# A kernel of attention and two MoE layers: V's local windows are loaded as runs of 112 keys

## The reference

```
# q, k, v: [4 batches, 8 heads, 576 tokens, 64]
q_d, k_d, v_d = means over groups of 4 tokens            # 144 tokens
out_up    = repeat(softmax(q_d k_d^T / 8) v_d, 4)        # pooled attention
mask      = |i - j| < 4                                  # a band of 7 keys
out_local = softmax(where(mask, q k^T / 8, -1e9)) v      # local attention
x = (out_up + out_local) as [2304 tokens, 512]
x = g(x @ w_in) @ w_out,    g = h * tanh(softplus(h))    # 512 -> 2048 -> 512
x = layernorm(h * softmax(h)) @ w_out2,  h = x @ w_in2   # 512 -> 1024 -> 512
```

## Time and profile before

| What | Value |
|---|---|
| Time, median of 3 runs | 689.77 us (688.67 to 690.86) |
| Span of the profiled execution | 686.9 us |
| The same execution's time beside the span | not recorded: the span is 2.9 us under the median of the runs |
| PE busy, share of the span | 667.5 us, 97% |
| DVE busy | 425.9 us, 62% |
| ACT busy | 326.0 us, 47% |
| POOL busy | 284.2 us, 41% |
| DMA packets | 26085, of them 12714 under 2 KB |

### The profile page before, as it was taken

The page is one execution under the profiler, slowest core; times in us unless marked ns, Lnnn a source line. Parts: engine busy times, 40 slices in busy tenths (PEclk is TensorE's granted clock), DMA queues, the critical chain, the costliest instruction groups (busy, mean ns, idle before and its releaser), DMA issues.

```text
span 686.9 us, 12938 instructions
## 1 busy us (share of the span) xinstructions
PE 667.5 (97%) x5002; PEld 573.1 (83%) x5002; DVE 425.9 (62%) x747; ACT 326.0 (47%) x687; POOL 284.2 (41%) x342
## 2 busy tenths in 40 slices
PE   6998899999999999999999999999999999999998
PEld 5777778888999989989899988888778888888886
DVE  7998759555765557555544412555788566766671
ACT  5998773233543446543443211137464454535441
POOL 6999713020694636645000000576435543354100
PEclk9999999999999999999999999999999999999999
DMA  8999692000000000000100001012100000000001
GB/s 259 247 262 262 157 336 114 0 1 1 0 1 1 1 1 1 1 1 1 62 1 2 1 0 35 27 31 63 31 17 16 31 32 31 8 25 31 32 16 46
DMA packets 26085, 37.52 MB, mean 55 GB/s; under 512 B 2484, under 2 KB 12714, under 8 KB 26026
## 3 DMA queue, kind: packets, MB, share of 16 engines
q1 hardware_dynamic: 26026, 36.71, 18.0%
HBM read 31.98 MB, written 4.72 MB: 53 GB/s over the span
## 4 chain that ended last, share of the span: by engine, by line
PE 89%; POOL 3%; DVE 2%; issue 2%; ACT 1%; DMA 1%; SPq 0%; POOLq 0%; DVEq 0%
PE psum L961 29%; PE psum L913 16%; PE psum L1074 13%; PE psum L1051 12%; PE psum L947 12%; PE psum L1060 2%; PE psum L813 1%; POOL prob L676 1%; PE psum L845 1%; PE psum L893 1%; DVE so L1768 1%; PE psum L832 1%; POOL half_qk L649 1%; DMA qkT<-kT_dram 1%; POOL half_v L659 1%
## 5 line engine op out<-in xcount | busy, mean ns | idle before, releaser
L961 PE MATMUL psum<-ghi,whi 128*128 128x512 f32 (+1 forms) x320 | 118.2, 370 | 0.0
L961 PE MATMUL psum<-glo,whi 128*128 128x512 f32 (+1 forms) x320 | 118.1, 369 | 0.0
L961 PE MATMUL psum<-ghi,wlo 128*128 128x512 f32 (+1 forms) x320 | 117.7, 368 | 0.0
L1210 ACT ACTIVATE g_sb<-psum 128x512 f32<-128x512 f32 (+1 forms) x48 | 25.3, 527 | 135.5 <-PE psum L913 134.7
L1586 DVE CAST ghi<-g_sb 128x512 fp32r<-128x512 f32 (+1 forms) x48 | 24.0, 500 | 101.8 <-PE psum L961 86.7
L913 PE MATMUL psum<-xhi,whi 128*128 128x512 f32 (+1 forms) x256 | 85.6, 365 | 0.5 <-ACT g_sb L1210 0.3
L1591 DVE TENSOR_TENSOR glo<-g_sb,ghi 128x512 fp32r<-128x512 f32 (+1 forms) x80 | 66.3, 829 | 19.6 <-ACT ghi L1236 17.9
L961 PEld LDWEIGHTS psum<-ghi,wlo 128*128 128x128 f32 x320 | 60.3, 189 | 10.2
L961 PEld LDWEIGHTS psum<-ghi,whi 128*128 128x128 f32 x320 | 60.5, 189 | 9.8 <-issue 0.4
L913 PE MATMUL psum<-xlo,whi 128*128 128x512 f32 (+1 forms) x192 | 68.0, 354 | 0.0
L961 PEld LDWEIGHTS psum<-glo,whi 128*128 128x128 f32 x320 | 60.5, 189 | 8.9
(11 more groups left out here) (175 smaller groups left out, 1618.7 us busy)
## 6 DMA issues: line engine op xcount, KB each, us to landing
wraw<-w_dram SPq DMA_DIRECT2D x12, 512.0 KB, 7.5
vw<-v_dram SPq DMA_DIRECT2D x30, 160.0 KB
qkT<-qT_dram SPq DMA_DIRECT2D x16, 288.0 KB, 4.0
qkT<-kT_dram SPq DMA_DIRECT2D x16, 288.0 KB, 5.7
out_dram<-ob SPq DMA_DIRECT2D x18, 256.0 KB, 2.0
v<-v_dram SPq DMA_DIRECT2D x16, 256.0 KB, 5.8
wraw<-w_dram SPq DMA_DIRECT2D x16, 256.0 KB, 6.8
b<-w_dram SPq DMA_DIRECT2D x4, 512.0 KB, 4.3
```

What stands on the lines that cost most here:

```text
L961: ins = nc.tensor.matmul(psum[:, YB + m, 0:size], a[:, w], b[:, (t * F1 + f) % GR, 0:size], start=(f == 0 and n == 0), stop=(f == F1 - 1 a ...
L1210: nc.scalar.activation(g_sb[:, f % HR, 0:size], psum[:, HB1 + f % HB, 0:size], ACT.Mish).then_inc(g_ok, 1)
```

## The change

Both blocks of a pair now take their keys from one run: partitions 0 to 111 of `vw` hold the 112 keys from the pair's first key on, in a row. Partitions 0 to 63 are the window of block 0, as before. Partitions 64 to 111 are keys 6 to 53 of block 1's window; partitions 112 to 121 (`P - OVER` = 122) are its keys 54 to 63, by a transfer of 10 rows; and partitions 122 to 127 are its keys 0 to 5, by a transfer of 6 rows, which are the six keys that block 0 has too. Block 1's keys are so rotated by six, and the subtraction that writes `prob` rotates its columns the same way: it is two instructions, one for columns 0 to 57 of each block, one for the last six. Unit 0 has five transfers into `vw` and unit 15 has four; the other 14 have three instead of two. `window_loads` counts accordingly. The bytes read and written for V are the same.

```diff
--- before.py
+++ after.py
@@ -404,8 +404,10 @@
 
         def window_loads(u):
 
-            return 2 * (u // 2 + 1) + (1 if u % 2 == 0 or u == UNITS - 1 else 0)
-
+            return 3 * (u // 2 + 1) + (2 if u % 2 == 0 else 1 if u == UNITS - 1 else 0)
+
+        RUN = 112
+        OVER = KW - QB
         LATE = 2
         FIRST = 2
         AHEAD = 4
@@ -528,18 +530,22 @@
 
 
 
-                for jp in range(2):
-                    i0, i1 = 0, NP
-                    if u == 0 and jp == 0:
-                        sp.dma_start(vw[SHIFT:KW, par, 0, :], v_u[0:KW - SHIFT]).then_inc(ld_vw[par], 16)
-                        i0 = 1
-                    if u == UNITS - 1 and jp == 1:
-                        i1 = NP - 1
-                        k0 = window(i1, 1)
-                        sp.dma_start(vw[KW:KW + SEQ - k0, par, i1, :], v_u[k0:SEQ]).then_inc(ld_vw[par], 16)
-                    src = bass.AP(v_u.tensor, v_u.offset + window(i0, jp) * P,
-                                  [[P, KW], [PSTEP * P, i1 - i0], [1, P]])
-                    sp.dma_start(vw[jp * KW:(jp + 1) * KW, par, i0:i1, :], src).then_inc(ld_vw[par], 16)
+                def rows(at, n, key, i0, i1):
+                    src = bass.AP(v_u.tensor, v_u.offset + (key + window(i0, 0)) * P,
+                                  [[P, n], [PSTEP * P, i1 - i0], [1, P]])
+                    sp.dma_start(vw[at:at + n, par, i0:i1, :], src).then_inc(ld_vw[par], 16)
+
+                i0, i1 = 0, NP
+                if u == 0:
+                    rows(16, RUN - 16, 16, 0, 1)
+                    rows(SHIFT, 16 - SHIFT, SHIFT, 0, 1)
+                    i0 = 1
+                rows(0, RUN, 0, i0, NP)
+                if u == UNITS - 1:
+                    i1 = NP - 1
+                    rows(RUN, SEQ - window(i1, 0) - RUN, RUN, i1, NP)
+                rows(RUN, P - OVER - RUN, RUN, 0, i1)
+                rows(P - OVER, OVER, QB, 0, NP)
 
             def load_w_in(c, kdx):
 
@@ -1495,9 +1501,13 @@
                 nc.vector.tensor_reduce(mx[:], scores, AX.X, ALU.max).then_inc(l_max, 1)
                 dve.wait_ge(l_max, u + 1)
                 wait(dve, l_turned, u - 1)
-                nc.vector.tensor_tensor(prob[:, par].rearrange("p i b k -> p b i k"), scores,
-                                        mx[:].unsqueeze(3).broadcast_to([P, 2, NP, KW]), ALU.subtract)\
-                  .then_inc(l_sub, 1)
+                to = prob[:, par].rearrange("p i b k -> p b i k")
+                for c0, c1, step in ((0, QB, OVER), (QB, KW, -QB)):
+                    turn = bass.AP(scores.tensor, scores.offset + c0,
+                                   [scores.ap[0], [scores.ap[1][0] + step, 2], scores.ap[2], [1, c1 - c0]])
+                    ins = nc.vector.tensor_tensor(to[:, :, :, c0:c1], turn,
+                                                  mx[:].unsqueeze(3).broadcast_to([P, 2, NP, c1 - c0]), ALU.subtract)
+                ins.then_inc(l_sub, 1)
 
             def sum_local(u):
                 par = u % 2
```

## The result

The changed kernel takes 686.28 us (median of 22 runs, 683.80 to 690.58), the kernel before 688.78 in the same number of runs. The ratio is 0.9964, with a 95% interval of 0.9951 to 0.9978: 2.5 us faster, where 2.6 had been forecast. The forecast started from 689.77, a median of three runs, 1.0 us over the median of 22 here. The profiled execution of the changed kernel was an ordinary one: 686.25 us with a span of 684.5. The two intervals have 0.9967 to 0.9978 in common, so the true gain is more likely 1.5 to 2.5 us than more.

A forecast was written before the change was run, and what follows sets the result against it. Attention decides: five resources nearly level, POOL leading, PE stopping for instructions. Terms -1.2 - 1.7 - 0.3 + 0.4 = -2.8 us took span 686.9 to 684.1; plus 2.9 gave 687.0, rounded up to 687.2 (range 685.6 to 691.4).

The forecast's parts named there:

- The mechanism: In attention, PE's stops within matmul runs are waits for its own next instructions behind crowded data; cheaper windows shorten them.
- the second rival: Window transfers in attention get no faster, since the 512-byte piece is slow: 690.4 us (689.6 to 691.5), chance 0.14.
- The term of the transfers: Attention's window transfers fall from 2.11 to 1.5 us a unit, all transfers of a unit from 4.75 to some 4.1.
- The bound "nothing gained": Slow end for a unit's window transfers in attention: they stay at 2.11 us; the other end was 0.98.
- The sum of the stops: Gains at PE's stops late in attention: -1.2 us for the stop itself and -1.7 for the slow clock behind it.
- -1.2 for half a stop: PE's 2.41 us stop near 76 us, at the end of attention, shrinks by half: -1.2 us.
- -1.7 for the clock: PE's clock no longer drops to 0.50 from 80.2 to 83.6 us, after the shorter stop: -1.7 us.
- DVE: Split subtraction in attention costs +0.14 us a unit, paid in three or so of 15 units: +0.4 us.
- the rival that DVE becomes the bound: Six-element rows cost +0.3 us a unit, so POOL waits for `rden` in nearly each: 692.5 us (691.9 to 693.5), chance 0.10.
- The -0.3 at **POOL: POOL's 0.91 us wait at 59.94 us, echo of PE's stop at 55, shrinks by a third: -0.3 us.
- SP: Issuing three window transfers instead of two takes SP +0.3 us a unit in attention, nothing on the path.
- The first rival: Window transfers get faster but nobody waits for them; PE's stop at 76.3 stays: 689.7 us (688.6 to 690.4), chance 0.33.

The follow-up runs named there:

- e5: Kernel before with 64 more wait instructions at the head of PE's list: 693.33 us, ratio 1.0061.
- e3: Kernel before with its two 64-row window transfers written to every second partition, output wrong: 685.35 us, ratio 0.9950.
- e4: Kernel before with window transfers for the first two units only, output wrong: 684.72 us, ratio 0.9935 to the kernel before.
- e6: Changed kernel's 112-row transfers with the single subtraction, without the 10- and 6-row transfers, output wrong: 684.46 us, ratio 0.9941 to the kernel before.
- e7: Kernel before with V's windows laid out again by the host, one 128-partition transfer of 2560-byte pieces per unit: 684.23 us, ratio 0.9931.
- e2: Changed kernel's transfers of 112, 10 and 6 rows with the single subtraction of before, output wrong: 687.21 us, ratio 0.9972 to the kernel before.
- e9: Kernel before unchanged, measured and profiled again: 688.80 us, ratio 0.9997.
- e1: Kernel before with only the subtraction split in two (580 and 60 elements), no rotation: 687.58 us, ratio 0.9980.
- e8: Kernel before with the subtraction in four instructions (460, 60, 60 and 60 elements): 689.34 us, ratio 1.0004.
- e10: Changed kernel unchanged, measured and profiled again (the second measurement): 687.02 us, ratio 0.9987 to the kernel before.
- e11: Kernel before with the first weight's four quarters requested in steps 4, 7, 10 and 13 instead of 13 to 16: 689.03 us, ratio 1.0001.

## Why the prediction was right, and where not

**The mechanism was right.** The time of attention is decided where PE stands still for its own instructions, behind crowded data. What had been a reading is now shown four ways: each long stop ends 1.35 to 1.77 us after a late packet of instructions has landed; the stops keep to one count modulo 256 in every profile; they move in the work when instructions are put ahead (e5); and with fewer or better placed window transfers they vanish and 4 us with them (e3, e4, e6, e7). The MoE layers take the same, as said. That the size came out within 0.1 us of the forecast is luck in part: the second measurement alone would have said 0.9 us, and two of the terms below were off.

Of the signs that the prediction named for being right, five came: a DMA share under 1 (0.91), two subtraction rows of 0.76 and 0.21 us, no stop over 1.5 us near 76, a granted clock of 1.00 from 80 to 85, and a first MoE matmul at 83.67 for 83.2. Two did not: the GB/s stayed at 255 from 30 to 65 us (260 for 255 from 10 to 76), which was the sign of the second rival, and POOL did not wait for `rden` at more places.

**The term of the transfers was mis-sized.** I had taken 1.5 us for a unit's windows instead of 2.11, so 4.1 us for a unit. Worked out as above, the transfers of the change keep the engines 4.27 to 4.35 us in three profiles, those of before 4.25 to 4.66 in five. The relief is between nothing and 0.4 us, about 0.1 by the means, and not 0.6; the 4.1 and less that I took is what e3 (3.98) and e7 (3.90) reach. The bound "nothing gained" was nearer than the middle.

**The sum of the stops was right by size, not by its parts.** -1.2 for half a stop and -1.7 for the clock were forecast. In the first pair of profiles the long stop is 0.8 shorter and the one of 1.00 is gone, 1.8 us together, and the slow clock behind a stop is still there after 1.62 us: a pause half as long was not what came. What the clock costs can be read from the same instructions in other profiles. The 120 PE instructions of before's slow stretch take 3.24 us, and 1.8 in e3, e6 and e7, so it cost 1.5; the 60 of the changed kernel's take 3.54 instead of 2.55, so 1.0 of it is still paid and 0.5 was won instead of 1.7. The clock fell to 0.50 behind stops of 1.39 (e2), 1.62, 1.77 (e9), 1.88 (e1), 2.13 (e8), 2.41, 2.69 (e10) and 3.73 us (e11), and not behind others of 1.64 (e1) and 1.42 (e10), so the length of a stop alone does not tell. That the total came out at -2.5 is an average over executions, which one profile of each kernel could not have given.

**DVE** costs +0.07 us in a unit instead of 0.14, and nothing measurable on the path; with it falls the rival that DVE becomes the bound, which e8 did not reach with three more instructions. Its price did not follow from its own rows either: with 0.27 us in hand, +0.3 leaves 0.03 in a unit, 0.4 us in 14 and not 2.8. The -0.3 at **POOL** was all that the sum had for the stop of 1.00 us, whose echo that wait was; the stop itself went in the first pair of profiles and had no term. **SP** costs nothing on the path, as said. The first rival, transfers that nobody waits for, is refuted by e3. The second, transfers that get no faster, was half true.

**What stays open.** Whether e1's 0.998 is more than scatter; what the narrow transfers cost; and why the run of 112 is so much less than every second partition. "DMA: Bandwidth & Descriptors", "Why a DMA increments its semaphore by 16 and not by 1", of the Trainium skill would put the 10 and 6 rows on 10 and 6 engines, an uneven load that could explain the second and part of the last; no view here shows single DMA engines. What else sets when a packet of instructions begins, so that it differs from execution to execution, is not known either.

## What to carry to other kernels

When PE is idle in the middle of a run with no releaser, count its instructions: if the places keep to one count modulo a fixed number, and a packet of the instruction queue lands shortly ahead of each, PE was waiting for instructions. Then cheaper or better spread data transfers help, although nothing waits for the data. Transfers into 64 partitions of one half kept the DMA engines busy longer here than the same rows on every second partition, so look for a layout in which each transfer is spread evenly over both halves; a run of 112 rows with two narrow transfers beside it won little of that. And where such stops are drawn anew in each execution, take many runs and compare their distributions: two profiles of one kernel differed by 2.4 us here, as much as the change is worth.

## What the runs showed of the hardware that was not expected

- PE's refills: a packet of 16,384 bytes for each 256 or so PE instructions. All 13 stops of over 1 us in attention that have no releaser lie at a count of 193 modulo 256 and end 1.35 to 1.77 us after the packet has landed.
- Waiting instructions on a semaphore that is already set, two waits in each, went through PE's list at one per 107 ns (e5: 61 of them from 1.6 to 8.1 us).
- Two subtractions on DVE without a wait between them overlap by 0.08 us (762 + 208 ns in 0.89 us, changed kernel).
- Spreading the same 64 rows over every second partition took the DMA engines' busy time for a unit's transfers from 4.25 to 4.66 us (five profiles) down to 3.98 (e3).
